# Global keys joined to a 96-key window, six key places, and softmax sums from a column of ones

## What is computed

```python
scores = scale * np.matmul(q, k.transpose(0, 1, 3, 2))
is_global = pos[None, :] < int(n_global)           # n_global = 8
is_local = (rel >= 0) & (rel < int(n_local))       # n_local = 96
bias = -slopes[:, None, None] * dist[None, :, :]
scores = np.where(is_global | is_local, scores + bias, -1e9)
a = np.exp(scores - scores.max(-1, keepdims=True))
a = a / (a.sum(-1, keepdims=True) + 1e-09)
x = np.matmul(a, v)                                # then [b, s, (h d)]
h = relu(x.T @ w_tok1) @ w_tok2;  u = x + h.T
x = u + relu(u @ w_ch1) @ w_ch2
theta = x @ w_theta
u = x + w_tok_r @ (x*cos(theta)) + w_tok_i @ (x*sin(theta))
out = u + relu(u @ w_ch)
```

## Time and profile before

| | |
|---|---|
| median of 3 runs | 528.64 us (528.63 to 528.68) |
| profiled execution | 529.02 us, of which span 527.2 us |
| PE busy | 509.6 us, 97% |
| PE weight loads busy | 475.3 us, 90% |
| DVE busy | 267.1 us, 51% |
| ACT busy | 181.8 us, 34% |
| POOL busy | 139.9 us, 27% |
| chain that ended last | PE 90%, DVE 6%, issue 2% |

### The profile page before, as it was taken

The page is one execution under the profiler, slowest core; times in us unless marked ns, Lnnn a source line. Parts: engine busy times, 40 slices in busy tenths (PEclk is TensorE's granted clock), DMA queues, the critical chain, the costliest instruction groups (busy, mean ns, idle before and its releaser), DMA issues.

```text
span 527.2 us, 8284 instructions
## 1 busy us (share of the span) xinstructions
PE 509.6 (97%) x3092; PEld 475.3 (90%) x3092; DVE 267.1 (51%) x671; ACT 181.8 (34%) x466; POOL 139.9 (27%) x129
## 2 busy tenths in 40 slices
PE   2999989999999999999999999999999999999997
PEld 2899889978999999987999999998888899888897
DVE  6888999845211232136211144327775584665452
ACT  4899889842111121113111123532223230331120
POOL 3555545339970000001300004550220130000040
PEclk9999999999999999999999999999999999999999
DMA  7754554403440000000300003140000011000002
GB/s 264 266 180 136 208 178 142 141 2 127 173 137 4 1 1 0 2 0 1 121 0 1 0 1 121 60 140 0 1 1 1 1 62 61 0 1 0 1 31 90
DMA packets 9258, 35.02 MB, mean 66 GB/s; under 512 B 1153, under 2 KB 3201, under 8 KB 7809
## 3 DMA queue, kind: packets, MB, share of 16 engines
q1 hardware_dynamic: 9216, 34.48, 19.1%
HBM read 31.33 MB, written 3.15 MB: 65 GB/s over the span
## 4 chain that ended last, share of the span: by engine, by line
PE 90%; DVE 6%; issue 2%; ACT 1%; DMA 1%; DVEq 0%; ACTq 0%
PE bank L271 70%; PE bank L1338 6%; PE bank L1121 5%; PE bank L1084 4%; PE bank L1102 2%; PE bank L1194 1%; DVE scores L855 1%; PE bank L1221 1%; DVE wsplit L770 1%; DVE wsplit L781 1%; PE bank L1149 1%; ACT probs L625 1%; DMA counts<-both_counts 1%; ACT probsT L579 0%; DVE act_raw L797 0%
## 5 line engine op out<-in xcount | busy, mean ns | idle before, releaser
L271 PE MATMUL bank<-hid,wsplit 128*128 128x384 f32 (+1 forms) x648 | 126.4, 344 | 0.1
L271 PEld LDWEIGHTS bank<-hid,wsplit 128*128 128x128 f32 x648 | 113.3, 188 | 3.9 <-issue 0.7
L271 PE MATMUL bank<-split,wsplit 128*128 128x384 f32 x576 | 108.1, 337 | 0.0
L271 PE MATMUL bank<-wsplit,zs 128*128 128x512 f32 (+1 forms) x576 | 104.1, 340 | 0.0
L271 PEld LDWEIGHTS bank<-wsplit,zs 128*128 128x128 f32 x576 | 89.1, 188 | 13.3
L271 PEld LDWEIGHTS bank<-split,wsplit 128*128 128x128 f32 x576 | 100.3, 188 | 0.0
L990 DVE SCALAR_TENSOR_TENSOR hid<-bank,hid 128x384 fp32r<-128x384 f32 x48 | 26.7, 557 | 140.4 <-ACT hid L704 140.4
L557 POOL TENSOR_TENSOR wsplit<-wraw,wsplit 128x1536 fp32r<-128x1536 f32 (+1 forms) x18 | 58.7, 3261 | 75.3 <-ACT wsplit L665 74.2
L704 ACT ACTIVATE hid<-bank 128x384 fp32r<-128x384 f32 x48 | 23.6, 491 | 143.8 <-PE bank L271 143.8
L556 POOL CAST wsplit<-wraw 128x1536 fp32r<-128x1536 f32 (+1 forms) x12 | 15.9, 1326 | 129.2 <-PE bank L271 123.0
L1084 PE MATMUL bank<-wsplit 128*128 128x232 f32 (+2 forms) x224 | 39.8, 310 | 10.0 <-DVE wsplit L830 9.0
(11 more groups left out here) (103 smaller groups left out, 534.5 us busy)
## 6 DMA issues: line engine op xcount, KB each, us to landing
wraw<-weights SPq DMA_DIRECT2D x16, 768.0 KB, 4.0
qk_raw<-qk SPq DMA_DIRECT2D x11, 1056.0 KB, 5.0
vt<-v SPq DMA_DIRECT2D x12, 256.0 KB, 3.2
out<-act_raw SPq DMA_DIRECT2D x16, 192.0 KB, 1.9
wraw<-weights SPq DMA_DIRECT2D x4, 512.0 KB, 3.5
qk_raw<-qk SPq DMA_DIRECT2D x1, 792.0 KB, 5.6
vg<-v_first SPq DMA_DIRECT2D x2, 256.0 KB, 5.6
qk_raw<-qk SPq DMA_DIRECT2D x1, 264.0 KB, 3.4
```

The costliest lines, as they stand in the source:

```text
L271: mm = pe.matmul(dst, lhs(a), rhs(c), start=first and i == 0, stop=last and i == 2, skip_group_check=True)
```

## The change

- The ring gets six places (`RING = T`), one for each tile of a batch, so that no window wraps. To make room, weight slot 5 is borrowed too and `probs` moves down by one slot.
- The 96 keys before the own tile and the 8 global keys are next to each other in the score row, and are now turned and weighed as one operand of 104 rows (`SEEN`), for all 128 queries. In units 0 and 6 that operand has only the 8 global keys. The separate global path (gather, transpose, copy, remainder, two wide matmuls, split global values) goes.
- The values come from the host with a column of ones per head (`VD = 65`), once as own tile and once as the 104 rows of the other operand; a unit's load is 128 x 1040 floats. Column 64 of each head's result is the sum of its probabilities, so the exponentials no longer accumulate.
- An output bank holds half a tile (4 heads, 260 columns). Sums are read (`read_sums`), inverted and multiplied for each half, 24 times in place of 12, at every odd step.
- `vt` has two places instead of three; several waits name other semaphores with the same sense. PE writes the identity into the banks for transposes before it starts.

```diff
-RING = 4
-PROBS_AT = 4
+RING = T
+PROBS_AT = 3
-BORROWED = 6
+BORROWED = 5
@@ sync
-                if n >= 3:
-                    sp.wait_ge(o_ready, n - 1)
-                sp.dma_start(vt[:, n % 3], v[b, t]).then_inc(v_in[n % 3], 16)
-                if t == 0:
-                    if b:
-                        sp.wait_ge(vg_lo, b)
-                    sp.dma_start(vg[:, :], v_first[b]).then_inc(vg_in, 16)
+                if n >= 2:
+                    sp.wait_ge(pv_done, PAIRS * (n - 1))
+                sp.dma_start(vt[:, n % 2], v[b, t]).then_inc(v_in[n % 2], 16)
@@ gpsimd
-            pool.wait_ge(gbias_ready, 1)
-            pool.memset(probs[:, :, :, 0:UNSEEN], 0.0).then_inc(unseen_ready, 1)
@@ scalar
-                act.activation(dst, src, ACT.Copy).then_inc(pT_taken, 1)
+                act.activation(probsT[:, m % 2], PT_BANK[m % 2][:, :], ACT.Copy).then_inc(pT_taken, 1)
-                if n >= 1 and p == 2:
-                    global_probsT(n - 1)
                         act.activation(probs[:, n % 2, h, first:], scores[:, m % 2, e, first:], ACT.Exp,
-                                       bias=nmax[:, n % 2, h:h + 1], scale=-1.0,
-                                       accum_out=psum[:, n % 2, h:h + 1]).then_inc(exp_done, 1)
+                                       bias=nmax[:, n % 2, h:h + 1], scale=-1.0).then_inc(exp_done, 1)
-                if p == 0 and n % T == 1:
-                    global_values_hi(n // T)
+                if g == 2:
+                    act.wait_ge(pv_done, STEPS)
@@ vector
+            def weighed(q):
+                return O_BANK[q % 2][:, 0:HALF_H * VD].rearrange("p (h d) -> p h d", h=HALF_H)
+
+            def read_sums(q):
+                dve.wait_ge(pv_done, 2 * (q + 1))
+                if q >= 2:
+                    dve.wait_ge(x_done, q - 1)
+                dve.tensor_scalar(rinv[:, q % 2].unsqueeze(2), weighed(q)[:, :, D:], 1.0e-9, None,
+                                  ALU.add).then_inc(sums_ready, 1)
+
+            def invert_sums(q):
+                dve.wait_ge(sums_ready, q + 1)
+                dve.reciprocal(rinv[:, q % 2], rinv[:, q % 2]).then_inc(rinv_ready, 1)
+
+            def take_x(q):
+                b, half = divmod(q, 2 * T)
+                dve.wait_ge(rinv_ready, q + 1)
+                dve.tensor_tensor(act_raw[:, b, half * HALF_H * D:(half + 1) * HALF_H * D].rearrange(
+                                      "p (h d) -> p h d", h=HALF_H),
+                                  weighed(q)[:, :, 0:D],
+                                  rinv[:, q % 2].unsqueeze(2).to_broadcast([P, HALF_H, D]),
                                   ALU.mult).then_inc(x_done, 1)
-                if p == 1 and n >= 1:
-                    gather(n - 1)
+                q = (m - 5) // 2 if m >= 5 and m % 2 else None
+                if q is not None:
+                    read_sums(q)
                 if n + 1 < UNITS:
                     queries_hi(n + 1, p)
+                if q is not None:
+                    invert_sums(q)
                 if 1 <= m <= STEPS - PAIRS:
                     keys_lo((m - 1) // PAIRS + 1, (m - 1) % PAIRS)
-                if p == 2 and n >= 1:
-                    global_probsT_lo(n - 1)
-                    invert_sums(n - 1)
-                if p == 0 and n >= 2:
-                    take_x(n - 2)
-                if p == 1 and n % T == 1:
-                    global_values_lo(n // T)
+                if q is not None:
+                    take_x(q)
@@ tensor, head_scores
+                if place == 0:
+                    first, key = P, 0
                 else:
-                    windows = [(UNSEEN, P, (RING - 1) * KW + G + UNSEEN), (P, WIN, 0)]
+                    first, key = UNSEEN, (place - 1) * KW + G + UNSEEN
@@ tensor, transpose_probs
+                keys = SEEN if n % T else G
                 for e in range(2):
+                    h, at = m % PAIRS * 2 + e, e * PT_HEAD
+                    pe.transpose(PT_BANK[m % 2][0:keys, at:at + P], probs[:, n % 2, h, OWN - keys:OWN],
+                                 ident[:, :])
+                    mm = pe.transpose(PT_BANK[m % 2][:, at + P:at + 2 * P], probs[:, n % 2, h, OWN:],
+                                      ident[:, :])
@@ tensor, weigh_values
+                if m % 2 == 0 and q >= 2:
+                    pe.wait_ge(x_done, q - 1)
+                keys = SEEN if n % T else G
                 for e in range(2):
+                    h, at = 2 * p + e, e * PT_HEAD
+                    cols = slice(h * VD, (h + 1) * VD)
+                    dst = O_BANK[q % 2][:, h % HALF_H * VD:(h % HALF_H + 1) * VD]
+                    pe.matmul(dst, probsT[:, m % 2, at + P:at + 2 * P], vt[:, n % 2, 0, cols],
+                              start=m % 2 == 0 and e == 0, stop=False, skip_group_check=True)
+                    mm = pe.matmul(dst, probsT[0:keys, m % 2, at:at + P], vt[0:keys, n % 2, 1, cols],
+                                   start=False, stop=True, skip_group_check=True)
@@ tensor, loop
+            for i in range(2):
+                for at in range(0, 2 * PT_HEAD, PT_HEAD):
+                    pe.transpose(PT_BANK[i][:, at:at + P], ident[:, :], ident[:, :])
```

More of the change, by code:

```diff
@@ L75, with build @@
 PI_IN = 3.1415925
-def build(nc, qk, v, v_first, both_counts, weights, out):
+def build(nc, qk, v, both_counts, weights, out):
     ctx = ExitStack()
@@ L185, in build @@
         qk_in = [sem(f"qk_in{i}") for i in range(2)]
-        v_in = [sem(f"v_in{i}") for i in range(3)]
+        v_in = [sem(f"v_in{i}") for i in range(2)]
         k_hi = sem("k_hi")
@@ L1082, in head_scores @@
                     for i in range(2):
-                        for first, last, key in windows:
-                            mm = pe.matmul(S_BANK[m % 2][e][:, first:last], q_split[:, n % 2, h, :],
-                                           k_split[:, i, h, key:key + last - first],
-                                           start=i == 0 and first == windows[0][0], stop=i == 1,
-                                           skip_group_check=len(windows) > 1)
+                        mm = pe.matmul(S_BANK[m % 2][e][:, first:WIN], q_split[:, n % 2, h, :],
+                                       k_split[:, i, h, key:key + WIN - first], start=i == 0, stop=i == 1)
                     mm.then_inc(s_ready, 1)
@@ L1381 @@
     first_keys = np.broadcast_to(kc[:, 0:1, :, :, 0:G], (B, T, D, H, G))
-    v_first = np.zeros((B, 2, H, G, H, D), v.dtype)
-    for h in range(H):
-        v_first[:, :, h, :, h] = v[:, None, h, 0:G]
+    rows = np.concatenate([v, np.ones((B, H, S, 1), v.dtype)], axis=3)
+    rows = rows.transpose(0, 2, 1, 3).reshape(B, T, P, H * VD)
+    v_rows = np.zeros((B, T, P, 2, H * VD), v.dtype)
+    v_rows[:, :, :, 0] = rows
+    v_rows[:, 0, 0:G, 1] = rows[:, 0, 0:G]
+    v_rows[:, 1:, 0:REACH, 1] = rows[:, :-1, UNSEEN:]
+    v_rows[:, 1:, REACH:SEEN, 1] = rows[:, 0:1, 0:G]
     def tiles(w):
```

154 lines of the change are left out of this document (32 added, 122 removed).

## The result

The changed kernel takes **602.71 us** (median of 4 runs, 597.63 to 602.89) against 528.64 us: ratio 1.138, 95% interval 1.133 to 1.143. It is 14% slower. 526.9 us was forecast, and no end of the range came near.

The account below looks back on a forecast made before the run. PE's own sequence was taken as the clock for warm attention units. Terms +1.95 + 0.2 - 3.04 + 0.2 + 0.4 - 0.2 - 0.6 - 0.1 - 0.5 = -1.7 us took 528.64 to 526.9 us, range 524.2 to 530.0.

Parts of the forecast that it names:

- First unit: Start of attention: eight-row operand adds PE work in unit 0; unit 2 begins at 28.4 instead of 26.44 us, +1.95.
- Rival (c): PE's clock rises at the same point of the work, not the same time: +1.6, 528.5 us; chance 0.10.
- Rival (d): Units 0 and 6: eight-row operands break PE's overlap, 32 switches at up to 0.22 us; 532 us at 0.2; chance 0.15.
- A step: PE's work on one pair of heads, warm: scores 0.50, transposes 0.44, values 0.87, together 1.81 us.
- Ordinary units: Warm attention units, four steps without global work: 7.24 us against 7.17, +0.07 each.
- Ring: Units 4 and 8: six places end the wrap, 8.76 becomes 7.24 us each, together -3.04; the one sure gain.
- Units 6 and 7: PE sets the pace: the pair costs at least 14.3 us, taken as 14.9, -0.6; DVE needs 13.2.
- The end: Attention from unit 11's first score: 12.0 us against 13.08; keeping half the stalls 12.6, -0.5.
- Stalls: Attention: collisions with POOL's long subtractions remain in part; unit 4 +0.2, unit 8 +0.4, unit 5 -0.2, unit 10 -0.1.
- rival (a): Attention's stalls go, as DVE and ACT lose work while PE's step grows: 524.5 us; chance 0.18.
- The collision: Attention: DVE casts beside POOL's long subtractions stay slow, 1.37 us against a mean of 0.33; sign: still over 1 us.
- DMAs: A unit's value load grows from 256 to 520 KB, about 5 us to land with 9 us available; effect nothing.

Follow-up runs that it names:

- unit 0 doubled: Kernel before the change with unit 0's transposes and value matmuls made twice, all of 128 rows; 534.38 us.
- full-rows form with dense matmuls: Changed kernel with 104 rows (96 of them zeros) in units 0 and 6, plus wide bfloat16 matmuls, result unused, in PE's waits at the start; 520.66 us.
- six places alone: Kernel before the change with only the ring of six key places, split global values in memory of their own; 526.16 us, ratio 0.9948.
- those of the widths: Second operand back to 96 queries in full-rows form: both 581.48, weighing 520.20, transposes 590.90 us; 128 in kernel before, unit 0 doubled, no wide matmuls: 548.92 us.
- three traces, at 22.7, 65.2 and 86.9 us: Changed kernel with, in order: dense matmuls first, 593.12 us; eight-row operand left out in unit 0 alone, 557.11; two wide matmuls a unit, 545.16.
- 8 of them: Changed kernel with 104 rows in units 0 and 6, plus eight dense matmuls in one place ahead of the first value weighing; 523.53 us.
- full-rows form: Changed kernel with 104 rows in units 0 and 6 too, 96 of them zeros, so no operand has eight rows; 596.16 us.

## Why the prediction was wrong

**The step that failed** is in "First unit": "If the clock rises at the same time, 25, the rest is warm". Everything behind it was priced at the upper level. I had both signs in the trace: the same instructions at double length ahead of 25 us, and a clock row that reads full all the same. I took the rise as an event in time. The runs show that it depends on the stream of instructions ahead of it, and the change rewrites that stream exactly there. Rival (c) let it come at the same point of the work, 3.2 us later; that mechanism exists (5.6 us later with unit 0 doubled), but I gave it a bounded price. No rival allowed that it might not come at all, which costs every later step its own length again: 13.57 - 7.11 = 6.5 us a unit. The right question was what PE would execute when it rises, and whether that stream would still raise it if it came later.

**Rival (d)** had the right place and the right price for its own part, and missed what it led to. I priced a switch at up to 0.22 us; it costs 0.19 at the lower level and 0.14 at the upper. Eight steps at 0.76 us are 6.1 us, and with full rows the kernel is 6.55 us faster. The rule of the Trainium skill ("TensorEngine Tiling (Array Packing)", section "Key Properties") that a change of tiling mode drains the engine fits, though the runs show a price and not a mode. That the clock falls in the same steps is the larger part, and was in no rival.

**What held once the level was up** is read from the full-rows form with dense matmuls.

- A step: 1.81 us forecast, 1.78 measured, 0.50 + 0.44 + 0.83. The value group is 0.83, the lower of my two bounds: I took 0.87.
- Ordinary units: 7.24 forecast; 7.11 measured without a wait, up to 7.31 with one.
- Ring: the run with six places alone gave 526.16, forecast at 526.2, with unit 8's loss of cover in place.
- Units 6 and 7: at least 14.3, "14.9 taken", 14.07 measured, with PE never idle by its record. DVE was busy for 12.3 of them, forecast 13.2.
- The end: 12.0 us floor, 12.6 taken; 11.9 measured (88.90 to 100.83).
- Stalls: I kept some 2 us; about 1 us is there, between my forecast and rival (a). Units 2 to 10 take 64.8 us, and PE's own need by my figures is 65.0, but that agreement is luck: my ordinary unit was 0.13 too long. By the measured lengths without a wait (eight units of 7.11, unit 6 of 6.96) the need is 63.8. The waits name what is left, PE's weight loads waiting for ACT's copy of the probabilities. Between 20 and 110 us there are six such waits, 1.0 us in all:

```profile
PEld bank L1074 <- ACT probsT L565: 1.0, 6, 0.2
```

- The collision: a cast beside POOL's long subtraction takes 0.89 us here instead of 1.37, below the 1 us that I had named as a sign. It is no cheaper. It starts 0.54 us into the subtraction and not 0.06, and it ends 0.15 us behind it in both kernels. The timelines of POOL and DVE:

```profile
44.71 1.28 POOL L503 TENSOR_TENSOR wsplit<-wraw,wsplit 128x512 fp32r<-128x512 f32 x1
...
45.25 0.89 DVE L750 CAST wsplit<-qk_raw 128x256 fp32r<-128x256 f32 x1
```

- DMAs: "nothing". Values landed in 3.8 us (median), and no unit waited for them.

Set against my forecast by stretches, unit 2 starts at 24.1 us instead of 28.4 (the earlier rise, -4.3), units 2 to 10 take 64.8 instead of 66.8 (-2.0), the end of attention 11.9 instead of 12.6 (-0.7), and the later layers 418.1 instead of 417.7 (+0.4). That is -6.6: from the forecast's span, 527.2 - 1.7 = 525.5 us, to the measured one, 518.9. The kernel as it was changed did not get there.

**What stays open.** Which property of a stream of small float32 instructions raises the level, holds it or loses it. The runs give cases on both sides, and I have no rule that sorts all of them. Most forms without a rise in attention, and those of the widths, ran once, and the moment of the rise differed by 2.5 us between two kernels with the same stream. So each of the widths' outcomes may be the form's or the execution's. Best supported are the falls within eight-row steps (three traces, at 22.7, 65.2 and 86.9 us) and the rise with dense matmuls and full rows (eight runs of two forms, all within 520.4 to 524.8 us). One of four runs of the changed kernel took 597.63 us instead of 602.7. It has no trace, and a stretch at the upper level is only a guess.

## What to carry to other kernels

Before you price a change to PE's work near its start, or after a phase of waits, find where durations halve in the trace and ask what the changed stream will be there. The level may not rise at all, and the loss is then that of the whole phase and not of the edit. Treat a clock column that reads full as unknown until it shows a change, and compare the durations of one instruction form instead. A few dense matmuls near a wait that exists anyway are a cheap test, and may be the cure: here 8 of them were worth 73 us. Avoid operands of eight rows between full ones; filled up with zero rows they cost less (3.39 us a step for 4.15). And run a form more than once before you say that its level does or does not rise.

## What was not expected of the hardware

- PE's clock fell without recorded idle time: at 22.7 and 65.2 us, in steps with eight-row value matmuls, after 6.7 and 44 us at the upper level. The switches' 0.14 us each count as busy there.
- The level depends on what came before. The same ordinary steps run at 1.78 us (upper, from 23 us to the end of attention) or at 3.39 us (lower, from 17.6 us to the end of attention in the full-rows form).
- A switch between operands of 128 and 8 rows costs 0.19 us at the lower and 0.14 us at the upper level. Operands of 104 and 128 rows alternate at no extra price (pairs of 0.43 us at the lower level, 0.22 at the upper).
- Eight-column transposes cost what 128-column ones do, 0.21 us at the lower level.
